# Bucket codes from six projection products per head instead of eight, with the high parts of q and k stacked in one tile and the low parts in another

## The reference, cut to what matters

```
q_bits = (einsum('bhsd,dk->bhsk', q, proj) > 0)         # 6 bits of each row of q
k_bits = (einsum('bhsd,dk->bhsk', k, proj) > 0)
q_bucket = sum(q_bits * 2 ** arange(6)); k_bucket = sum(k_bits * 2 ** arange(6))
mask = q_bucket[:, :, :, None] == k_bucket[:, :, None, :]
scores = where(mask, q @ k.T / 8, -1e9)
attn = exp(scores - max) / (sum + 1e-9);  x = attn @ v  # 2 x 8 heads, 768 rows, 64 columns
x -> (a = x @ w1) * (b = x @ w2) @ w3 @ w_out           # 1536 tokens
out = sum over 4 experts of p[e] * (relu(x @ w1[e]) @ w2[e])
```

## Time and profile before

| | |
|---|---|
| median of 3 runs | 1009.63 us (1008.54 to 1010.49) |
| the profiled execution | 1008.62 us |
| its span, first to last instruction | 1006.8 us |
| granted TensorE clock, mean | 1.0 (2.4 GHz) |
| PE, PEld busy | 990.4 us (98%), 921.5 us (92%) |
| DVE, ACT, POOL busy | 636.6 us, 461.3 us, 412.2 us |
| PE in the projections (L1343), 128 matmuls of 384 columns | 32.8 us |
| DMA queue, share of 16 engines over the span | 20.1% |

### The profile page before, as it was taken

How to read it: one execution, slowest core, us unless ns; L and a number is a source line. 1 busy time by engine, 2 the same in 40 slices (tenths; PEclk the granted TensorE clock), 3 DMA queues, 4 the chain that set the end, 5 groups by cost and what they waited for, 6 DMA issues and landing times.

```text
span 1006.8 us, 15884 instructions
## 1 busy us (share of the span) xinstructions
PE 990.4 (98%) x5504; PEld 921.5 (92%) x5504; DVE 636.6 (63%) x963; ACT 461.3 (46%) x853; POOL 412.2 (41%) x416
## 2 busy tenths in 40 slices
PE   7999999999999999999999999999999999999998
PEld 6879999999988999999998998989989899898997
DVE  5349899999996997398865353453634536345342
ACT  3338888888786544354452150421504225042230
POOL 4022334285457993494355160341603416043130
PEclk9999999999999999999999999999999999999999
DMA  6323333333332221011020110201102011010102
GB/s 241 95 71 95 95 104 108 102 101 87 97 94 80 63 64 42 22 43 43 1 64 21 42 43 1 63 21 43 43 1 62 21 42 42 11 52 21 42 16 109
DMA packets 58925, 60.58 MB, mean 60 GB/s; under 512 B 7808, under 2 KB 46848, under 8 KB 58880
## 3 DMA queue, kind: packets, MB, share of 16 engines
q1 hardware_dynamic: 58880, 60.00, 20.1%
HBM read 44.20 MB, written 3.19 MB: 47 GB/s over the span
## 4 chain that ended last, share of the span: by engine, by line
PE 90%; DVE 5%; issue 2%; ACT 2%; DMA 1%; POOL 0%; SPq 0%; DVEq 0%; ACTq 0%; POOLq 0%
PE ps L288 23%; PE ps L289 22%; PE ps L290 22%; PE ps L1378 6%; PE ps L1365 3%; PE ps L1367 3%; PE ps L1391 3%; PE ps L1393 3%; PE ps L1343 2%; PE ps L1338 2%; DVE w_lo L1016 1%; DVE hid_lo L1138 1%; DVE pT_lo L1001 1%; PE ps L1300 1%; DMA w_raw<-in_moe_w 1%
## 5 line engine op out<-in xcount | busy, mean ns | idle before, releaser
L615 POOL TENSOR_TENSOR v_sum<-kept,kept 128x384 f32<-128x384 f32 x48 | 52.2, 1088 | 291.9 <-ACT kept L796 291.9
L1270 DVE SCALAR_TENSOR_TENSOR acc<-ps,gate,acc 128x512 f32<-128x512 f32 x96 | 72.0, 750 | 134.7 <-PE ps L290 134.7
L796 ACT COPY kept<-ps 128x384 f32<-128x384 f32 x144 | 64.3, 480 | 200.6 <-PE ps L290 200.0
L290 PE MATMUL ps<-v_hi,hid_lo 128*128 128x512 f32 x384 | 149.6, 390 | 0.0
L289 PE MATMUL ps<-v_lo,hid_hi 128*128 128x512 f32 x384 | 149.5, 389 | 0.0
L288 PE MATMUL ps<-v_hi,hid_hi 128*128 128x512 f32 x384 | 149.4, 389 | 0.0
L983 DVE TENSOR_SCALAR_CACHE_REDUCE expo<-ps 128x768 f32<-128x768 f32 x96 | 91.6, 954 | 15.3 <-PE ps L1367 14.9
L703 ACT ACTIVATE expo<-expo,neg_max 128x768 f32<-128x768 f32 x96 | 90.6, 944 | 6.5 <-DVE expo L983 5.0
L1257 DVE SCALAR_TENSOR_TENSOR hid_lo<-c,hid_hi 128x384 fp32r<-128x384 f32 x96 | 64.4, 683 | 46.1 <-ACT hid_hi L917 19.1
L711 ACT CAST pT_hi<-ps 128x768 fp32r<-128x768 f32 x96 | 76.7, 801 | 32.2 <-PE ps L1378 31.9
L1001 DVE TENSOR_TENSOR pT_lo<-ps,pT_hi 128x768 fp32r<-128x768 f32 x96 | 90.3, 945 | 1.5 <-ACT pT_hi L711 1.5
(11 more groups left out here) (157 smaller groups left out, 2509.0 us busy)
## 6 DMA issues: line engine op xcount, KB each, us to landing
w_raw<-in_moe_w SPq DMA_DIRECT2D x64, 128.0 KB, 2.4
e_raw<-in_moe_w SPq DMA_DIRECT2D x64, 128.0 KB, 2.3
v_raw<-in_moe_w SPq DMA_DIRECT2D x32, 256.0 KB, 3.0
w_raw<-in_moe_w SPq DMA_DIRECT2D x8, 512.0 KB, 4.1
raw_q<-in_q SPq DMA_DIRECT2D x16, 192.0 KB, 2.9
raw_k<-in_k SPq DMA_DIRECT2D x16, 192.0 KB, 3.0
raw_v<-in_v SPq DMA_DIRECT2D x16, 192.0 KB, 2.7
q_main<-q_cross SPq DMA_DIRECT2D x16, 192.0 KB, 2.7
```

The source lines that it names most:

```text
L290: return nc.tensor.matmul(out_ps, lhs_lo, rhs_hi, start=False, stop=stop, skip_group_check=onto)
L615: nc.gpsimd.tensor_tensor(v_sum[:, :], kept[s][1][:, :], kept[s][2][:, :], ALU.add).then_inc(v_done, 1)
L796: nc.scalar.copy(kept[s][n][:, :], ps[4 * s + n][:, 0:HALF]).then_inc(kept_done, 1)
L1270: nc.vector.scalar_tensor_tensor(acc[:, t, :], ps[4 * ((h + t // 4) % 2) + t % 4], gate_f[:, bass.ds(t * E + e, 1)], acc[:, t, :], ALU.mul ...
```

## The change

`high_parts` holds q high in columns 0 to 63 and k high in 64 to 127, `low_parts` holds k low, then q low. Their transposes go to `highs` and `lows`, which are single tiles, used by every head in turn. The projection is six matmuls: for each half of the rows `highs` with two weight tiles (high and low part of proj, on both q and k rows) and `lows` with one. `q_cross` and `k_cross` no longer come from ACT; SP moves their four halves from `highs` and `lows` by DMA. So `move_high` (2 DMAs) becomes `move_parts` (6 DMAs). Since `highs` and `lows` have no second buffer, ACT's first copy of a head waits until the six moves of the head before have landed (`parts_moved`). The one-hots have a semaphore of their own. POOL makes both high parts first, then both low parts.

```
-            def move_high(m, s):
+            def move_parts(m, s):
                 sp.wait_ge(prep_copied, 4 * m + 4)
-                move(s, (q_main[s][0:DH, :], q_cross[s][0:DH, :]), (k_main[s][0:DH, :], k_cross[s][DH:P, :]))
+                move(parts_moved[s], (q_main[s][0:DH, :], highs[0:DH, :]), (k_main[s][0:DH, :], highs[DH:P, :]),
+                     (q_cross[s][0:DH, :], highs[0:DH, :]), (k_cross[s][DH:P, :], highs[DH:P, :]),
+                     (q_cross[s][DH:P, :], lows[DH:P, :]), (k_cross[s][0:DH, :], lows[0:DH, :]))
...
             for s in range(2):
-                move_high(s, s)
+                move_parts(s, s)
                 move_onehots(s, s)
...
-            def prep_copy(m, s, j):
+            def prep_copy(m, i, s, j):
+                if j == 0 and s:
+                    act.wait_ge(parts_moved[0], 96 * (i + 1))
+                elif j == 0 and (not isinstance(i, int) or i):
+                    act.wait_ge(parts_moved[1], 96 * i)
                 act.wait_ge(prep_mm, GROUPS * m + j + 1)
-                dst = (q_cross if j < 2 else k_cross)[s]
                 half = slice((j % 2) * HALF, (j % 2 + 1) * HALF)
-                nc.scalar.copy(dst[:, half], ps_prep[:, 0:HALF]).then_inc(prep_copied, 1)
+                nc.scalar.copy((highs if j < 2 else lows)[:, half], ps_prep[:, 0:HALF]).then_inc(prep_copied, 1)
...
                 elif j == 4:
                     for n, w in enumerate(proj_w):
-                        half = slice((n // 4) * HALF, (n // 4 + 1) * HALF)
-                        last = nc.tensor.matmul(ps_prep[:, 0:HALF], w[:, :],
-                                                (q_cross if n % 4 < 2 else k_cross)[s][:, half],
-                                                start=n == 0, stop=n == 7)
+                        half = slice((n // 3) * HALF, (n // 3 + 1) * HALF)
+                        last = nc.tensor.matmul(ps_prep[:, 0:HALF], w[:, :], (lows if n % 3 == 1 else highs)[:, half],
+                                                start=n == 0, stop=n == 5)
...
                 if t == 0:
-                    pe.wait_ge(stacks_moved[s], 64 * (i + 1))
+                    pe.wait_ge(parts_moved[s], 96 * (i + 1))
+                    pe.wait_ge(onehots_moved[s], 32 * (i + 1))
```

More of the change, by code:

```diff
@@ L176, in build_program @@
         raw_k = [place(f"raw_k{s}", [P, TILES, DH], F32, prep_at) for s in range(2)]
-        q_parts = [place(f"q_parts{s}", [P, TILES, P], F32R, prep_at) for s in range(2)]
-        k_parts = [place(f"k_parts{s}", [P, TILES, P], F32R, prep_at) for s in range(2)]
-        proj_w = [place(f"proj_w{n}", [P, P], F32R, prep_at) for n in range(8)]
+        high_parts = [place(f"high_parts{s}", [P, TILES, P], F32R, prep_at) for s in range(2)]
+        low_parts = [place(f"low_parts{s}", [P, TILES, P], F32R, prep_at) for s in range(2)]
+        proj_w = [place(f"proj_w{n}", [P, P], F32R, prep_at) for n in range(6)]
         onehot = place("onehot", [P, S], F32R, prep_at)
@@ L188, in build_program @@
             k_main[s] = place(f"k_main{s}", [P, S], F32R, prep_at)
+        highs, lows = (place(n, [P, S], F32R, prep_at) for n in ("highs", "lows"))
         assert prep_at[0] <= rec_at[0] - S * 4
@@ L233, in build_program @@
         v_loaded = [sem(f"v_loaded{n}") for n in range(2)]
-        stacks_moved = [sem(f"stacks_moved{n}") for n in range(2)]
+        parts_moved = [sem(f"parts_moved{n}") for n in range(2)]
+        onehots_moved = [sem(f"onehots_moved{n}") for n in range(2)]
         w_loaded = [sem(f"w_loaded{n}") for n in range(RAWS)]
@@ L466, in held, with split_highs @@
                 pool.sem_inc(pool_held, 1)
-            def split_q(m, i, s, first):
+            def split_highs(m, i, s, first):
                 if not first:
@@ L505, in _ @@
             nc.gpsimd.memset(ident[:, :], 0.0).then_inc(zeros_set, 1)
-            for n in range(8):
+            for n in range(6):
                 nc.gpsimd.memset(proj_w[n][:, :].bitcast(F32), 0.0).then_inc(zeros_set, 1)
@@ L734, in copy @@
                         if not last:
-                            prep_copy(m + ahead, (s + ahead) % 2, j)
+                            prep_copy(m + ahead, i + (s + ahead) // 2, (s + ahead) % 2, j)
                     def lower(ahead, hf):
@@ L1058, in constants @@
                 dve.wait_ge(const_loaded, 16 * (4 + B))
[L1059 removed]
+                dve.wait_ge(zeros_set, 7)
                 nc.vector.tensor_copy(code[:, :, :], code_f[:, :, :]).then_inc(code_ready, 1)
[L1061 to L1068 removed]
+                q_rows, k_rows = slice(0, DH), slice(DH, P)
+                for h in range(2):
+                    q_cols, k_cols = (slice(c, c + BITS) for c in (DH * h, DH * h + KBIT))
+                    for n, rows, cols in ((0, q_rows, q_cols), (0, k_rows, k_cols), (1, k_rows, q_cols), (1, q_rows, k_cols)):
+                        nc.vector.tensor_copy(proj_w[3 * h + n][rows, cols], proj_f[rows, :]).then_inc(proj_hi_ready, 1)
+                dve.wait_ge(proj_hi_ready, 8)
+                for h in range(2):
+                    q_cols, k_cols = (slice(c, c + BITS) for c in (DH * h, DH * h + KBIT))
+                    for rows, cols in ((q_rows, q_cols), (k_rows, k_cols)):
+                        nc.vector.tensor_tensor(proj_w[3 * h + 2][rows, cols], proj_f[rows, :],
+                                                proj_w[3 * h][rows, cols].bitcast(F32), ALU.subtract)\
+                            .then_inc(proj_ready, 1)
                 nc.vector.reduce_sum(dp_sum[:, :], dp[:, :, :], axis=AX_X).then_inc(gate_step, 1)
@@ L1331, in prep @@
                 if j == 0:
+                    pe.wait_ge(q_hi_done, m + 1)
+                    pe.wait_ge(k_hi_done, m + 1)
+                if j == 2:
                     pe.wait_ge(q_split, m + 1)
-                if j == 2:
                     pe.wait_ge(k_split, m + 1)
                 if j < 4:
-                    parts = (q_parts if j < 2 else k_parts)[s]
+                    parts = (high_parts if j < 2 else low_parts)[s]
                     for tt in range(HT):
```

49 lines of the change are left out of this document (22 added, 27 removed).

## The result

| | before | after |
|---|---|---|
| median | 1009.58 us, 6 runs (1008.54 to 1010.49) | 1038.88 us, 6 runs (1034.12 to 1040.04) |
| the profiled execution | 1008.62 us | 1038.12 us |
| its span | 1006.8 us | 1036.3 us |

The ratio of the runs is 1.0282, 95% interval [1.0269, 1.0294]: 29 us slower, where 3.5 were forecast. The direction and the places were right; both sizes were too small, one of them by far.

What follows compares the result with a forecast made beforehand. The prediction took PE, busy 98% of the span, as the bound: -5.6 (projections) + 4.3 (stage 1) + 4.8 (loop) = +3.5 us, so 1012.1 us own time, 1013.1 as a median, with an 8 in 10 range of 1006.5 to 1026.5.

Steps and rivals of the forecast that it cites:

- PE's saving: Two projections fewer in each of 16 heads, 32 matmuls at 0.175 us: 5.6 us off PE, gained at once.
- The stop in stage 1: ACT's first copy of head 1 waits for head 0's moves, w3's high part behind it; PE loses 4.3 us.
- loss of clock: PE's clock falling after its 3.6 us pause in stage 1: taken as none, 2.3 us kept for the range.
- The stop in the loop: Attention: four added moves per head delay the one-hots, PE waits 0.53 us in 9 slots, +4.8 us.
- The price of 2.9 for the landing: Attention loop: the second one-hot move lands 2.9 us after its issue, as in the profile before.
- X: Landing of a slot's second one-hot move, counted from B: forecast 12.15 us; PE waits if it exceeds 11.62.
- B: Start of SP's first move of high parts in an attention slot, 172.71 us in the profile before.
- The count of slots: Attention slots in which PE would wait for the one-hots: 9 ordinary ones, at 0.53 us each.
- Rival 1: Loop moves cost only their issue, so PE never waits there: -1.3 us, 1008.3 as a median; chance 0.22.
- rival 4: Head 0's moves land before PE needs the copy and the loop hides all: -5.6, 1004.0 median; chance 0.05.
- Rival 2: The loop's queue backs up, X goes towards 13.9: +23.7 us, 1033; chance 0.12.
- Rival 3: PE loses its clock in the stop of stage 1: +2.3 us on the forecast, 1015.4; chance 0.11.

Runs made afterwards that it cites:

- experiment 6: The kernel before with the two projections per head that multiply low weights with k_cross left out, six matmuls instead of eight: 1006.03 us, ratio 0.9956 to before.
- experiment 7: version 3 with DVE's small operation `guarded` (adding 1e-9 to a head's row sums) left out: 1003.43 us, ratio 0.9937 to before.
- version 3: The changed kernel with head 0's moves issued between the loads of w3 and the read back put behind the one-hot moves: 1008.51 us, ratio 0.9982 to before.
- experiment 1: The changed kernel with head 0's six moves issued between the loads of w3 instead of after the last: 1029.96 us, ratio 1.0196 to before.
- experiment 5: The changed kernel with the read back, from the third head on, cut to 48 of 768 columns, in its old place: 1027.29 us, ratio 1.0161 to before.
- experiment 4: The kernel before with four more moves per head of 196,608 bytes each, into two spare tiles nobody reads: 1035.26 us, ratio 1.0256 to before.

## Why the prediction was wrong, step by step

**PE's saving: right in size, paid out only in part.** -5.6 us of PE work; ordinary slots without stops are 15.06 us, as worked out (experiments 6 and 7). But PE was not the only bound. The profile of before said so in the rows I used, DVE with 13.8 to 15.5 us in slots of 15.2 to 16.5. A saving on PE of 5.6 us was worth 4.2 us in experiment 6 and 2 in version 3. This error is 1.4 to 4 us and on the optimistic side. POOL's new order, which I had cost at nothing, is part of it: `guarded` grew from 0.64 to 0.78 us on average by what POOL does beside it.

**The stop in stage 1: right mechanism, +4.3 forecast, 6.0 us measured.** From `multiply_wp(4)` to `multiply_wp(5)` it is 54.51 - 41.53 = 12.98 us, where before has 47.43 - 40.44 = 6.99. Two terms were too small. The stage ran 1.09 us later than in before (`multiply_wp(4)` at 41.53 and not 40.44, the wait for the load of w3 under experiment 1); with that added, the first move landed to the tenth where it should, but the moves landed 0.85 us apart and not 0.75, the last one 1.35 behind the fifth, so the copy came at 51.07 and not at 50.1. And I took no loss of clock: PE stood still for 4.36 us instead of 3.6 and came back at the lower level, which cost 1.45 us. That term belonged into the sum, if not with all of the 2.3 us that I had kept for the range.

**The stop in the loop: the step that failed.** It is the term "the read back's own data is now right in front of them in the queue; I take 0.05 for it". It measured 1.0 us (experiment 5), in thirteen slots. The price of 2.9 for the landing was read where 2.3 us lay between the issue of the read back and that of the one-hots; I moved the one-hots right behind it and kept the price. X was 13.45, not 12.15, and the wait 13.55 - 11.62 = 1.93 us and not 0.53. The rest of that chain, B + 8.1 for the landing of the store and 8.7 for the one-hots, stood. Of the 1.3 us that X was off, 1.0 is the read back's data, 0.15 the issue of the one-hots; 0.2 is left in their landing, 3.1 behind a small read back where before has 2.9.

**The count of slots: wrong too.** I let three long slots hide X, and two others have it below the bound; slot 13 is in both groups, so the forecast's own count is 10 and not 9. With X at 13.45 nothing hides: of the thirteen slots the shortest are 15.9 and 16.8 us. 13 x (1.93 - 0.35) = 20.5 us, and the thirteen slots grew by 223.55 - 201.98 = 21.6. That is close partly by chance. The last slot is 1.1 us shorter than the ordinary 17.0, the two long slots of before add nothing to theirs, and against that two slots are longer, 17.94 and 19.84 us. The longer one had PE idle for 2.93 us for the one-hots, and then, by stretches of 2 us (columns as above),

```profile
150.00:152.00 2.00, 0.49 (x4) 0.17 (x2) 1.28 (x2) 1.60 (x4) 0.20 (x1) 1.00 0.94 247
...
154.00:156.00 2.00, 2.00 (x10) 1.91 (x9) 0.97 (x2) 0.50 (x2) 0.51 (x1) 0.50 0.00 0
156.00:158.00 2.00, 2.00 (x15) 2.00 (x13) 1.14 (x3) 1.25 (x2) 0.56 (x1) 0.71 0.00 0
```

half the clock for 2 us and less than full for 2 more. The usual stops of 1.46 to 1.95 us left the clock at 1.00 in this execution, and so did the 2.61 us in the slot of 17.94.

**The rivals.** Rival 1 (the queue keeps up) and rival 4 are refuted by the trace. The rule of the Trainium skill that I weighed (DMA: Bandwidth & Descriptors, "Where 436 GB/s comes from") would have a move at 0.45 us; here the six land 0.85 us apart in the loop, 231 GB/s, slower even than the 0.75 that I took from stage 1. Another section of the Trainium skill (SBUF — State Buffer, "Door 1: The DMA port swizzle") says that 64 partitions that start at 0 or 64 reach only eight of the sixteen ports and gives about 218 GB/s as the limit of such a transfer. By that a move of 196,608 bytes would take 0.90 us, an estimate from that page. It is much the nearer of the two, but the runs are faster than this limit as well: 0.85 us in the loop, 231 GB/s, and 262 GB/s by the spacing of the four landings in stage 1 of the kernel before. Rival 2 is the nearest: its X of 13.9 for 13.45 measured, its 1033 for 1038.88. It had argued a queue that is slow as a whole, though, and the landing grew by one term that stood in my own sum with 0.05 beside it. Rival 3 happened, at 1.45 us for its 2.3.

**The range.** Its upper end stood in the middle of the case that came true. Two unknown costs, the landing behind a read back and the clock after a pause, each had a bound that the trace gave (+25 and +2.3 us), and I cut the range at half of the first.

## What to carry to other kernels

In a queue that one engine feeds in order, a price for a landing holds only for the traffic that stood in front of it where it was read; when a change moves a transfer right behind another of the same size, add that transfer's own time (here 1.0 us). A wait for a store in the middle of that engine's program (store, wait, read back) makes everything behind it late by all that is in front of it, so put what another engine waits for ahead of it: here two reorderings of SP's program were worth 30 us, where the change takes 5.6 us off PE. And a slot in which two engines are within a microsecond of each other can give back less than what is taken from one of them, even where the profile calls the first one 100% busy (experiments 6 and 7).

## What the runs showed of the hardware

- Moves of 64 partitions (196,608 bytes), issued every 0.64 us, land 0.85 us apart: in the loop B + 2.7 for the first and B + 3.06 + 3.9 for the sixth, so 4.3 us for five. A landing took 2.7 us for the first of six and 3.9 us for the sixth, and 5.6 us in stage 1, where a load of 512 KB was ahead. The store of 3 KB behind them took 3.0 us instead of 2.4.
- After a pause of PE the granted clock fell in some cases and not in others, and the length of the pause does not tell which. It stayed at 1.00 behind pauses of 1.95 and 2.61 us in the changed kernel and of 2.32 in experiment 1. Stretches at 0.50 followed pauses of 2.93 and 4.36 us in the changed kernel, of 2.35 in experiment 1, of 2.62 and 1.84 in experiment 5, and of 1.80 in experiment 4. One of each kind, the first from the changed kernel, the second from experiment 4 (the matmul behind the pause, then a stretch of 2 us behind it):

```profile
135.16 0.43 PE L1385 MATMUL ps<-k_main,q_main 128*128 128x384 f32 x1 [2.61 <-DMA k_main<-onehot]
136.00:138.00 2.00, 2.00 (x20) 2.00 (x19) 1.36 (x3) 1.47 (x3) 1.13 (x2) 1.00 0.00 0
```
```profile
112.12 0.44 PE L1375 MATMUL ps<-k_main,q_main 128*128 128x384 f32 x1 [1.80 <-DMA k_main<-onehot]
114.00:116.00 2.00, 2.00 (x11) 2.00 (x10) 1.15 (x5) 1.30 (x3) 0.47 (x1) 0.50 0.04 8
```

- Once or twice in most executions, between 95 and 145 us, an issue on SP took 0.9 to 1.7 us where its neighbours take 0.60 or less; the kernel before has one too (1.36 us at 96.14). Where the one-hots have slack it costs nothing; in the changed kernel's slots of 17.94 and 19.84 us it was one of the six moves (1.56 and 1.28 us), and the read back went out at B + 8.9 and B + 9.4. Why it happens is open.
- The lock between DVE and POOL, shown under experiment 7. Leaving the DVE operation out shows what it costs; that POOL's operation is what holds it rests on the ends of the rows, since no run moved POOL's work away from it.
